# Unread products behind the memory products and behind the routed tiles' logits

## The reference, cut to what matters

```python
# attention with a memory: B, H, S, D = 4, 8, 576, 64
local = softmax(q @ k.T / sqrt(D), causal) @ v
q_p = where(q > 0, q, exp(q) - 1) + 1
mem_out = (q_p @ M_prev) / (q_p @ z_prev + 1e-06)
g = sigmoid(beta)
x = g * mem_out + (1 - g) * local            # to 2304 tokens x 512
# routed layer: 8 experts, 512 -> 1024 -> 512
logits = x @ w_gate
expert_idx = argmax(logits); gate_w = softmax(logits)[expert_idx]
x[e] = gate_w * relu(x[e] @ w1[e]) @ w2[e]   # tokens of expert e
# dense layer: 512 -> 2048 -> 512
h = x @ w_in
out = where(h > 0, h, exp(min(h, 0)) - 1) @ w_out
```

## Time and profile before

| | us |
|---|---|
| median of 3 runs | 1227.66 |
| the profiled execution | 1224.04 |
| its span, first to last instruction | 1222.3 |
| TensorE busy | 1149.7 (94%) |
| VectorE busy | 618.7 (51%) |
| ScalarE busy | 417.7 (34%) |
| GpSimd busy | 240.1 (20%) |
| granted TensorE clock, mean | 0.93 of full |

### The profile page before, as it was taken

One profiled execution on the slowest core, in us unless ns is written; L12 is line 12 of the kernel. 1 busy time (PEld: TensorE's weight loads), 2 busy tenths in 40 slices (PEclk: granted clock), 3 DMA queues, 4 the chain that ended last, 5 costly groups with the idle time before them and its releaser, 6 DMA issues.

```text
span 1222.3 us, 20912 instructions
## 1 busy us (share of the span) xinstructions
PE 1149.7 (94%) x6508; PEld 995.9 (81%) x6509; DVE 618.7 (51%) x1282; ACT 417.7 (34%) x853; POOL 240.1 (20%) x158
## 2 busy tenths in 40 slices
PE   5999999899999997998998998789999999999998
PEld 4887878788898776777886887579998999989997
DVE  4676686568665745446227226434342443434332
ACT  3454454344344303334126115322222323222222
POOL 1121332233133224126007106430000000000000
PEclk8899898788876979999999999889999999999999
DMA  5244227133622329437017215410000000000000
GB/s 119 61 99 150 60 61 185 49 85 94 173 60 53 97 75 318 139 112 249 34 43 256 96 43 172 164 52 26 27 27 26 0 26 26 26 26 1 27 1 26
DMA packets 48215, 102.72 MB, mean 84 GB/s; under 512 B 14992, under 2 KB 19088, under 8 KB 48144
## 3 DMA queue, kind: packets, MB, share of 16 engines
q1 hardware_dynamic: 38336, 79.51, 22.3%
q10 hardware_dynamic: 6768, 12.32, 3.0%
q0 software_dynamic: 3040, 9.96, 2.7%
HBM read 81.84 MB, written 19.94 MB: 83 GB/s over the span
## 4 chain that ended last, share of the span: by engine, by line
PE 64%; issue 21%; POOL 6%; DVE 4%; DMA 3%; ACT 1%; SPq 1%; ACTq 1%; DVEq 0%; POOLq 0%
PE ps L707 17%; PE ps L720 16%; PE ps L524 8%; POOL wparts L411 5%; PE ps L482 4%; PE ps L507 4%; PE ps L531 4%; PE ps L499 3%; PE ps L484 3%; PE ps L659 2%; DMA kraw<-kT 2%; PE ps L547 1%; PE ps L539 1%; PE ps L487 1%; PE ps L692 1%
## 5 line engine op out<-in xcount | busy, mean ns | idle before, releaser
L707 PE MATMUL ps<-th,wparts 128*128 128x384 f32 x768 | 198.5, 339 | 4.6 <-ACT orow L953 3.1
L720 PE MATMUL ps<-wparts,gh 128*128 128x512 f32 x576 | 179.4, 392 | 0.0
L707 PEld LDWEIGHTS ps<-th,wparts 128*128 128x128 f32 x768 | 142.3, 190 | 12.9 <-issue 3.9
L1030 DVE TENSOR_REDUCE negmax<-ps 128x1 f32<-128x128 f32 (+4 forms) x160 | 86.7, 542 | 118.8 <-PE ps L487 116.4
L524 PE MATMUL ps<-vbuf,probT 128*128 128x64 f32 (+1 forms) x960 | 137.8, 291 | 5.5 <-DVE xrow L1068 3.0
L524 PEld LDWEIGHTS ps<-vbuf,probT 128*128 128x128 f32 (+1 forms) x960 | 122.4, 205 | 18.7 <-DVE probT L1041 8.2
L707 PE MATMUL ps<-tl,wparts 128*128 128x384 f32 x384 | 130.4, 339 | 0.0
L801 ACT ACTIVATE prob<-ps,negmax 128x128 f32<-128x128 f32 (+4 forms) x160 | 91.2, 570 | 110.0 <-PE ps L507 98.7
L636 PE MATMUL ps<-wparts,xh 128*128 x368 | 116.9, 399 | 12.0 <-DVE xl L1218 9.2
L659 PE MATMUL ps<-wparts,hh 128*128 x352 | 115.1, 409 | 8.7 <-POOL wparts L411 2.8
L720 PEld LDWEIGHTS ps<-wparts,gh 128*128 128x128 f32 x576 | 106.6, 188 | 18.3
(11 more groups left out here) (175 smaller groups left out, 1886.1 us busy)
## 6 DMA issues: line engine op xcount, KB each, us to landing
stage<-weights SPq DMA_DIRECT2D x52, 512.0 KB, 4.9
stage_first<-weights SPq DMA_DIRECT2D x28, 512.0 KB, 4.7
qraw<-qT SPq DMA_DIRECT2D x32, 288.0 KB, 4.3
kraw<-kT SPq DMA_DIRECT2D x32, 288.0 KB, 5.2
xs<-x_sorted ACTq DMA_DIRECT2D x24, 256.0 KB, 2.7
y_slots<-yrow ACTq DMA_DIRECT2D x23, 256.0 KB, 2.1
qpair<-qT SPq DMA_DIRECT2D x32, 144.0 KB, 2.9
out<-orow SPq DMA_DIRECT2D x18, 256.0 KB, 2.1
```

The lines of the kernel that those rows point to most:

```text
L707: mm = nc.tensor.matmul(ps[:, H_B[f % 2], 0:GN], wparts[:, at:at + P], x[:, r, c, :], start=c == 0 and x is th and part == 0, stop=c == DC ...
L720: mm = nc.tensor.matmul(ps[:, j, :], x[:, f % RING, P * j:P * j + P], wparts[:, at:at + D], start=f == 0 and x is gh and part == 0, stop=f ...
L1030: nc.vector.tensor_reduce(negmax[:, k % 4:k % 4 + 1], scores_row(k)[:, 0:KV[k % QT]], AX_X, ALU.max, negate=True).then_inc(max_done, 1)
```

## The change

`stay_busy` moves up in the file, unchanged. `memory` calls it with 2 behind each of its first four products, in every head of every batch. `batch` calls it with 6 behind the logits of each of the routed tiles inside the batches; the tiles of the last batch, routed behind the loop, are as before.

```diff
+            def stay_busy(count):
+
+                for _ in range(count):
+                    nc.tensor.matmul(ps[:, BO, SPARE_COLUMN:].rearrange("p (i d) -> p i d", i=2), ident_r[:],
+                                     ident_r[:, 0:(BANK - SPARE_COLUMN) // 2].unsqueeze(1)
+                                     .to_broadcast([P, 2, (BANK - SPARE_COLUMN) // 2]), start=True, stop=True)
+
             def memory(b, n, prev):
...
                     mm = nc.tensor.matmul(memory_out()[0:rows, i, :], qphi[half, P * i:P * i + rows],
                                           mzbuf[half, m % 2, :], start=True, stop=True)
+                    if i < QT - 1:
+                        stay_busy(2)
                 mm.then_inc(mem_done, 1)
...
                     if tile is not None:
                         logits(b - 1, tile)
+                        stay_busy(6)
```

More of the change, by code:

```diff
@@ L526, in weigh @@
                 mm.then_inc(pv_done, 1)
[L528 to L533, removed]
             def turn_routed(b, i, bank):
```

## The result

The changed kernel takes 1360.32 us (median of 4 runs, 1343.67 to 1365.88) against 1225.27 of the kernel before (4 runs); the ratio is 1.105, 95% interval 1.085 to 1.126. The forecast was no change, 1225, with a range of 1207 to 1248. The profiled execution took 1354.91 us, its span is 1353.2. Executions of one kernel differ by up to some three per cent, and the ratios here compare the faster executions of both kernels.

What follows compares the result with a forecast made beforehand. TensorE was taken as the bound in the four attention batches, with 120 of 402 us lost to the lower clock. +42.4 + 3 - 2.9 - 36.6 - 5.1 = +0.8 us gave 1225 us, range 1207 to 1248.

Steps and rivals of the forecast that it cites:

- (a): Unread products between memory products: 256 at 0.1225 us each at full clock, 31.4 us.
- (f): Clock in the attention: denser light stretches give back 36.6 us behind memory products and 5.1 at batch ends.
- (b): Six unread products behind each routed tile's logits in three batches: 90 in all, 11.0 us.
- (c): Sum of the added products: 42.4 us (36.7 to 44.6), and 3 us more for those at the lower clock.
- (d): At three batch ends the added products fill part of TensorE's waits for a softmax row: -2.9 us.
- (e): Memory products' semaphore reaches ScalarE's exponential 1 us later: zero cost, at most a part of 15.7 us.
- Rivals 1, 2 and 4: Clock doesn't answer, 1275 us (chance 0.08); it answers half, 1253 (0.15); later exponential holds up softmax rows, 1241 (0.04).
- rule on idle gaps: Clock drops come from TensorE's idle gaps, so products added where it has none keep no clock; same 1275 us.

Runs made afterwards that it cites:

- order-only kernel: Against the kernel before: four unread products ahead of the memory products moved one each behind the first four of them, nothing added; 1328.55 us, ratio 1.094.
- full-height kernel: Against the kernel before: memory products on all 128 rows, the memory matrix's other half zero, no added product; 1186.7 us, ratio 0.979.
- full-height kernel with pairs: Against the kernel before: memory products on 128 rows, two unread products behind each of the first four, nothing behind the logits; 1198.51 us, ratio 0.987.
- kernel with half-height pairs: Against the kernel before: two unread products on 64 rows behind each of the first four memory products, nothing behind the logits; 1282.98 us, ratio 1.047.
- block on 128 rows: Against the kernel before: eight unread products on 128 rows in one block behind the fifth memory product, nothing behind the logits; 1236.4 us, ratio 1.0039.
- block on 64 rows: Against the kernel before: eight unread products on 64 rows in one block behind the fifth memory product, nothing behind the logits; 1297.48 us, ratio 1.066.

## Why the prediction was wrong

**Two steps failed, (a) and (f).** The attention grew by 130 us more than forecast. By the count above 126 of them are the clock, step (f) (42 us expected back, 84 lost), and the rest is work. But (f) was built on (a): the change of height, which (a) put at nothing, is all that the order-only kernel adds, and that kernel lost 103 us by the clock.

**Step (a)** is the price of a product between memory products, bounded by 0.106 and 0.129 us. It was 1.94 / 8 = 0.24 us at full clock. I bounded it by rows in which products of one kind follow each other, and the price lay in the change of kind. The trace of before had it, in a row that I did not weigh:

```profile
62.78 0.65 PE L531 MATMUL ps<-ident_r 128*128 128x152 f32 x4
```

Four unread products that start at 62.78, with the memory products of 63.37 behind them, take 0.59 us; with scores behind them 0.49. The edit makes eight more changes of height in each head. In its stretch they cost 1.94 - 0.91 (the eight at equal height: 2.14 - 1.23 us in the full-height kernels with and without pairs) = 1.03 us, 0.13 for each. The queue of weight loads shows it too. Loads of the changed kernel, then those of the full-height kernel with pairs, and the matmuls that belong to the latter:

```profile
58.37 0.29 PEld L506 LDWEIGHTS ps<-mzbuf,qphi 64*128 64x128 f32 x2
58.73 0.30 PEld L493 LDWEIGHTS ps<-ident_r 128*128 128x128 f32 x2
```

```profile
53.90 0.30 PEld L506 LDWEIGHTS ps<-mzbuf,qphi 128*128 128x128 f32 x2
54.12 0.30 PEld L494 LDWEIGHTS ps<-ident_r 128*128 128x128 f32 x2
...
55.40 0.19 PEld L506 LDWEIGHTS ps<-mzbuf,qphi 128*64 128x64 f32 x2
```

```profile
53.97 0.37 PE L506 MATMUL ps<-mzbuf,qphi 128*128 128x65 f32 x2
54.15 0.43 PE L494 MATMUL ps<-ident_r 128*128 128x152 f32 x2
```

At equal height a load starts 0.03 to 0.07 us ahead of its matmul, under the product before; at a change of height it starts with it (58.37 and 58.37, 58.73 and 58.73). A change in the columns alone does the same: the last memory product of the full-height kernel uses 64 columns, its load starts with it (55.40 and 55.40), and the two unread products ahead of it take 55.40 - 55.04 = 0.36 us, where two of them take 53.97 - 53.70 = 0.27 in the middle.

The Trainium skill (TensorE: Matmul & The Clock Gate, "Part 3: Packing small matmuls — row/col tiling") has a weight load pulled ahead of running matmuls where its row group does not conflict with theirs, or where it goes into the background weight buffer; its list of what overlaps has only the first. Loads of 64 rows behind products of 128 share rows with them, and they didn't overlap. But loads of all 128 rows behind products of all 128 did, which the list as written excludes, and so did loads of 64 rows behind products on the same 64 (67.37 against the matmul's 67.40 in the kernel with half-height pairs). Why a change of height or width stops the overlap, no run shows.

**Step (f) had the wrong sign.** I expected 37 us back, and 5 at batch ends; 84 were lost. It rested on the picture that more columns make the lightest part denser. With the switches it became longer and emptier (21 matmuls where there had been 29): the order alone, without one product added, brought 206 us more of low clock. And more columns do not help by themselves: eight products on 64 rows, with no switch more, brought 120 us more. That unread products behind the memory products can give clock back was right: the block on 128 rows is near the edit that I had in mind, and it came out at 1.004, near the forecast for the edit that was made. That the emptiness of the stretch is what lowers the clock is not shown: it fits the order-only kernel, but the block on 64 rows is nearly as full as the one on 128 (1.05 us for the same eight products against 0.96) and loses clock all the same. What the runs show is that changes of height and products on half the rows each lower it.

**Point by point.** (b) The sixes: 172.44 - 171.73 = 0.71 us for six, 0.118 each, as put; what they were to give back did not show (1.0099 in time, 12 us in all).

```profile
171.73 0.88 PE L493 MATMUL ps<-ident_r 128*128 128x152 f32 x6
172.44 0.32 PE L482 MATMUL ps<-khl,qhi 128*128 128x256 f32 x1
```

(c) The sum at full clock is 1.94 x 32 + 0.118 x 90 = 73 us instead of 42. At the low clock a head's memory stretch is 5.42 us, from 218.42 to 223.84, against 2.30 in the kernel before (second fence): 3.12 more, less than twice 1.94, since a switch does not double (3.12 less 8 x 0.23 leaves 1.28 us for eight). That explains in part why the 73 us, less 11 of waits, appear as only 46 in the account above, which takes all work to double; the rest is open, within the two digits of the clock or not.

```profile
218.42 0.69 PE L506 MATMUL ps<-mzbuf,qphi 64*128 64x65 f32 x2
219.04 0.71 PE L493 MATMUL ps<-ident_r 128*128 128x152 f32 x2
...
223.84 0.69 PE L482 MATMUL ps<-khl,qhi 128*128 128x384 f32 x1
```

```profile
379.65 2.37 PE L499 MATMUL ps<-mzbuf,qphi 64*128 64x65 f32 x10
381.95 0.69 PE L482 MATMUL ps<-khl,qhi 128*128 128x384 f32 x1
```

(d) The waits at batch ends are gone, as the view of TensorE's waits shows; only the one in the first steps is left of the four of the earlier trace rows. (e) held: no new wait for softmax rows. Two slips in the prediction changed nothing: the stretch at full clock that it calls the first of the earlier trace rows is the one from 303.88, and the lower end of its own range comes to 1215 by its terms, not 1213.

```profile
PE ps L482 <- DVE qlo L1006: 12.3, 1, 12.3
PE ps L482 <- ACT prob L804: 2.9, 1, 2.9
PE ps L482 <- issue: 1.3, 1, 1.3
```

Rivals 1, 2 and 4 had the right sign; the first went furthest, to 1275 us. It let the clock stay as it was, and none let the clock get worse. The rule on idle gaps that the prediction cites from the Trainium skill (TensorE: Matmul & The Clock Gate, "Why this matters for your kernels") isn't what decides here: TensorE was busy 534.9 of 537.9 us and the clock fell more than before, and in the full-height kernel, with idle time of 371.5 - 355.9 = 15.6 us, a third of it in one gap of 5.2, it fell less.

## What to carry to other kernels

Price an inserted instruction by the pair it forms with its neighbours, on both sides, not by rows in which its own kind repeats. Look first whether the rows and columns of the array that it uses are theirs. Where a stretch of small products costs the clock, give those products the full height (zeros in the other half cost no time here: 1.23 us against 1.29) before adding products that nobody reads; and give unread products the full height too. An experiment that only moves what is there, and adds nothing, tells order from amount in one run.

## What the runs showed of the hardware

- A change between products on 64 and on 128 rows of the array takes 0.13 us at the full clock (1.03 us for eight) and, by an estimate, 0.16 at the lower one (1.28 for eight), in a chain of float32 products of 128-column weights; the weight load then starts with its matmul and not ahead of it. At a change from 128 to 64 columns it does too, and the two products ahead took 0.09 us more.
- Eight products on 64 rows hold TensorE's clock less than the same on 128 rows: 0.75 against 0.86 over the attention, 1.066 against 1.004 in time, and less than none (0.85).
- A busy share says nothing of this: TensorE was busy 534.9 of 537.9 us in the attention of the changed kernel, at a clock of 0.73.
